# An FFT convolution followed by two MLPs: the second half of a scratch buffer read back in two partition ranges on two queues, and one product moved ahead

## The reference

```python
X = np.fft.rfft(x, axis=1)                 # x: (2, 3008, 256) float32
Y = X * (filt_r + 1j * filt_i)[None]
y = np.fft.irfft(Y, n=3008, axis=1)        # tokens: 2 * 3008 = 6016 rows of 256
h = y.reshape(6016, 256) @ w1_in           # 256 -> 2048
z = np.maximum(0.01 * h, h) @ w1_out       # 2048 -> 256
h = z @ w2_in
r = np.maximum(h, 0.0)
out = (r * r) @ w2_out                     # (6016, 256)
```

## Time and profile before

| | us |
|---|---|
| median of 3 runs | 1065.8 (1065.09 to 1067.39) |
| the profiled execution's own time | 1064.64 |
| its span | 1062.5 |
| PE busy | 1057.0 |
| DVE busy | 827.9 |
| ACT busy | 563.3 |
| POOL busy | 316.1 |

### The profile page before, as it was taken

One profiled execution on the slowest core, in us unless ns is written; L12 is line 12 of the kernel. 1 busy time (PEld: TensorE's weight loads), 2 busy tenths in 40 slices (PEclk: granted clock), 3 DMA queues, 4 the chain that ended last, 5 costly groups with the idle time before them and its releaser, 6 DMA issues.

```text
span 1062.5 us, 13988 instructions
## 1 busy us (share of the span) xinstructions
PE 1057.0 (99%) x5120; PEld 879.8 (83%) x5120; DVE 827.9 (78%) x1142; ACT 563.3 (53%) x979; POOL 316.1 (30%) x287
## 2 busy tenths in 40 slices
PE   9999999999999999999999999999999999999998
PEld 9558888888888888888999888888888888888998
DVE  2877898887887887787887886887887887786666
ACT  3667564564554654555554554644554554454543
POOL 1995654434343343341321211220220220210000
PEclk9999999999999999999999999999999999999999
DMA  9696000121112112112344000100100100100100
GB/s 316 176 304 231 10 1 17 36 52 46 51 49 49 52 47 51 52 33 55 118 152 147 21 1 1 40 1 1 40 1 1 40 1 1 40 1 1 40 1 35
DMA packets 66724, 61.45 MB, mean 58 GB/s; under 512 B 40688, under 2 KB 53856, under 8 KB 66656
## 3 DMA queue, kind: packets, MB, share of 16 engines
q1 hardware_dynamic: 66160, 60.06, 18.2%
q10 hardware_dynamic: 496, 0.49, 0.1%
HBM read 36.55 MB, written 23.99 MB: 57 GB/s over the span
## 4 chain that ended last, share of the span: by engine, by line
PE 98%; DMA 1%; SPq 0%; DVE 0%; ACT 0%; issue 0%; ACTq 0%
PE PS L1046 16%; PE PS L1047 16%; PE PS L1048 16%; PE PS L1054 14%; PE PS L1055 14%; PE PS L1056 14%; PE PS L935 2%; PE PS L959 2%; PE PS L1002 1%; PE PS L1022 1%; PE PS L979 1%; DMA X<-in_x 0%; DMA zu<-U 0%; DMA V<-zu 0%; SPq L219 0%; PE PS L999 0%
## 5 line engine op out<-in xcount | busy, mean ns | idle before, releaser
L683 ACT ACTIVATE GH<-GF 128x512 fp32r<-128x512 f32 (+1 forms) x384 | 238.7, 622 | 295.3 <-DVE GF L878 154.4
L884 DVE TENSOR_TENSOR GL<-GF,GH 128x512 fp32r<-128x512 f32 (+1 forms) x384 | 273.7, 715 | 110.4 <-ACT GH L683 103.7
L1048 PE MATMUL PS<-GH,WOL 128*128 128x512 f32 (+1 forms) x768 | 295.8, 385 | 0.0
L1047 PE MATMUL PS<-GL,WOH 128*128 128x512 f32 (+1 forms) x768 | 295.8, 385 | 0.0
L1046 PE MATMUL PS<-GH,WOH 128*128 128x512 f32 (+1 forms) x768 | 295.8, 385 | 0.0
L1054 PE MATMUL PS<-XH,WIH 128*128 128x512 f32 (+1 forms) x672 | 259.5, 386 | 0.0
L1056 PE MATMUL PS<-XH,WIL 128*128 128x512 f32 (+1 forms) x672 | 258.8, 385 | 0.0
L876 DVE SCALAR_TENSOR_TENSOR GF<-GF 128x512 f32<-128x512 f32 (+1 forms) x192 | 167.5, 913 | 1.6
L1048 PEld LDWEIGHTS PS<-GH,WOL 128*128 128x128 f32 x768 | 144.2, 188 | 27.0
L1046 PEld LDWEIGHTS PS<-GH,WOH 128*128 128x128 f32 x768 | 144.2, 188 | 26.8
L1047 PEld LDWEIGHTS PS<-GL,WOH 128*128 128x128 f32 x768 | 144.2, 188 | 26.6
(11 more groups left out here) (85 smaller groups left out, 941.9 us busy)
## 6 DMA issues: line engine op xcount, KB each, us to landing
V<-zu SPq DMA_DIRECT2D x12, 512.0 KB, 5.9
zu<-U SPq DMA_DIRECT2D x31, 192.0 KB, 3.7
out_y<-YT SPq DMA_DIRECT2D x5, 1024.0 KB, 4.3
X<-in_x SPq DMA_DIRECT2D x8, 512.0 KB, 8.9
FL<-in_filt SPq DMA_DIRECT2D x16, 224.0 KB, 5.0
wi<-PWH SPq DMA_DIRECT2D x16, 224.0 KB, 2.5
wi<-PWL SPq DMA_DIRECT2D x16, 224.0 KB, 3.1
WIH<-wi SPq DMA_DIRECT2D x8, 448.0 KB, 3.4
```

The lines of the kernel that those rows point to most:

```text
L683: nc.scalar.activation(GH[:, g, 0:width(s)], GF[:, g, 0:width(s)], ACT.Copy).then_inc(g_hi[kind], 1)
L884: nc.vector.tensor_tensor(GL[:, g, 0:w], GF[:, g, 0:w], GH[:, g, 0:w].bitcast(f32), ALU.subtract).then_inc(g_lo[kind], 1)
L1047: nc.tensor.matmul(acc, wh, xl, start=False, stop=False)
L1048: return nc.tensor.matmul(acc, wl, xh, start=False, stop=last)
```

## The change

The reads of V[0] stay as they are. The six reads of V[1] become six others, over three pieces of 4, 8 and 12 residues. Partitions 0 to 95 of each piece (the "body"; frequencies of units 8 to 13) are read by ACT's queue, from a place behind `y_copy(4)` and `x_round0(1)`, once units 11, 12 and 13 are stored. Partitions 96 to 127 (the "rest"; units 14 and 15) are read by SP's queue behind the last three stores, where the six reads stood. Sequences 12 and on wait for both parts of their piece: 12 and 13 for the first, 14 to 17 for the second, 18 to 23 for the third. And `up_1(1)` moves from behind `up_5(0)` to the place behind `up_1(0)`, in front of sequence 12.

```diff
+V_PIECES = ((0, 4), (4, 12), (12, 24))
+V_BODY = 96
...
+            def load_v_rest(n):
+                a, b = V_PIECES[n]
+                by_js = zu[1].rearrange("j s m e -> (j s) m e")
+                sp.dma_start(V[1][V_BODY:, a:b, :, :].rearrange("p m b d -> p m (b d)"), by_js[V_BODY:, a:b, :]).then_inc(v_rest[n], 16)
...
             for n in range(UNITS - RINGS, UNITS):
                 sp.wait_ge(*stored(n))
-            for g in range(MH // 4):
-                load_v(1, g)
+            for n in range(len(V_PIECES)):
+                load_v_rest(n)
...
+            def load_v_body(n):
+                a, b = V_PIECES[n]
+                by_js = zu[1].rearrange("j s m e -> (j s) m e")
+                act.dma_start(V[1][0:V_BODY, a:b, :, :].rearrange("p m b d -> p m (b d)"), by_js[0:V_BODY, a:b, :]).then_inc(v_body[n], 16)
+
             for c in Y_ACT:
                 if DRAIN[-1] <= c < 14:
                     y_copy(c)
                 if c == 4:
                     x_round0(1)
+                    for n in range(UNITS - 2 - RINGS, UNITS - 2):
+                        act.wait_ge(z_out[n % RINGS], 32 * (n // RINGS + 1))
+                    for n in range(len(V_PIECES)):
+                        load_v_body(n)
...
-                pe.wait_ge(v_in[half][g], 16)
+                if half == 0:
+                    pe.wait_ge(v_in[g], 16)
+                else:
+                    piece = [a <= 4 * g < b for a, b in V_PIECES].index(True)
+                    pe.wait_ge(v_body[piece], 16)
+                    pe.wait_ge(v_rest[piece], 16)
...
             up_1(0)
+            up_1(1)
             for c in range(CH, 19):
                 sequence(c)
...
             for s in range(1, SLOTS):
-                up_1(s)
-                if s == 1:
+                if s > 1:
+                    up_1(s)
+                else:
                     sequence(22)
                 up_2(s)
```

More of the change, by code:

```diff
@@ L117, in fft_mlp_kernel @@
         z_out = [sem(f"z_out{r}") for r in range(RINGS)]
-        v_in = [[sem(f"v_in{h}{g}") for g in range(MH // 4)] for h in range(2)]
+        v_in = [sem(f"v_in{g}") for g in range(MH // 4)]
+        v_body = [sem(f"v_body{n}") for n in range(len(V_PIECES))]
+        v_rest = [sem(f"v_rest{n}") for n in range(len(V_PIECES))]
         y_ps = sem("y_ps")
@@ L249, in stored, with load_v @@
                 return z_out[i % RINGS], 32 * (i // RINGS + 1)
[L251 to L254, removed]
+            def load_v(g):
+                by_js = zu[0].rearrange("j s m e -> (j s) m e")
+                sp.dma_start(V[0][:, 4 * g:4 * g + 4, :, :].rearrange("p m b d -> p m (b d)"),
+                             by_js[:, 4 * g:4 * g + 4, :]).then_inc(v_in[g], 16)
+            def load_v_rest(n):
+                a, b = V_PIECES[n]
+                by_js = zu[1].rearrange("j s m e -> (j s) m e")
+                sp.dma_start(V[1][V_BODY:, a:b, :, :].rearrange("p m b d -> p m (b d)"), by_js[V_BODY:, a:b, :]).then_inc(v_rest[n], 16)
             for b in range(B):
@@ L277, in _ @@
                 if 0 <= i - NU < MH // 4:
-                    load_v(0, i - NU)
+                    load_v(i - NU)
             for n in range(UNITS - RINGS, UNITS):
                 sp.wait_ge(*stored(n))
-            for g in range(MH // 4):
-                load_v(1, g)
+            for n in range(len(V_PIECES)):
+                load_v_rest(n)
             sp.wait_ge(p_ps, 4 * UNITS)
```

## The result

Median of six runs 1073.05 us (1071.83 to 1075.51) against 1065.44 before (1064.16 to 1067.39, six runs): ratio 1.0072, 95% interval [1.006, 1.0083]. The change costs 7.6 us where "no difference" was forecast, and lies outside the range. The profiled execution took 1074.45 around a span of 1072.3.

A forecast was written before the change was run, and what follows sets the result against it. PE was taken to bound the kernel, with one 1.33 us hole before sequence 12. 1.33 - 0.05 = 1.3 us gained from the median of 1065.8 gave 1064.5 us, range 1063.3 to 1066.8.

The forecast's parts named there:

- What bounds the kernel, and the size of the hole: PE holds 98% of the span; its one wait, before sequence 12 for V, is 1.33 us, all this edit can bring.
- Edit 1: up_1(1) in front of sequence 12 runs inside the hole: worth 0.70 us even if V comes no sooner.
- Edit 2a: First rest on SP behind the last stores: lands 2.7 us after issue (2.1 to 3.84), at 85.6, before 86.14.
- Edit 2b: Body on ACT, issued at 80.00, delays the stores in SP's queue by 0 to 0.8 us, taken as 0.1.
- Edit 2c: Three body issues in ACT's queue take 1.43 us and free ACT 0.96 late; no cost to PE.
- Edit 2d: Third piece of V, wanted by sequence 18 at 91.5, lands at 91.0 to 91.9: no wait, above 0.4 us.
- ACT held up: Rival: three slow issues free ACT at 85.6, delaying y_copy(6) and up_2(0); time 1066.5 us, chance 0.09.
- What is late next: Behind the hole, up_7(1) waits 0 to 0.1 us for whole_c(0), taken as 0.05; no other PE wait.
- The rule: Skill's advice against splitting by partition halves, since transfers serialize: V would land no sooner, at 86.72, gain 0.70 us.
- Only the order counts: Rival: the first rest comes as late as the old piece, V at 86.7; gain 0.7, time 1065.1, chance 0.26.
- The slow one: Rival: third piece lands at 93 to 95, sequence 18 waits 1.5 to 3.5 us; 1067.5 at 94.5, chance 0.13.

The follow-up runs named there:

- e4: Changed kernel with V[1] in six pieces of four residues, only the first split between ACT and SP, the others whole on SP; ratio to before 0.9987.
- e11: The same kernel as e4, measured once more on another chip: 1063.91 us against 1065.36, ratio 0.9982.
- e6: Kernel before with up_1(1) in front of sequence 12 and each SP read of V[1] cut in 96 and 32 partitions; ratio to before 1.0009.
- e2: Changed kernel without the body: SP reads all 128 partitions of the three pieces behind the last stores; ratio to before 1.0005.
- e3: Changed kernel with six pieces of four residues in place of three, body on ACT, rest on SP; ratio to before 1.0057.
- e5: Five foreign reads: kernel before with up_1(1) moved, ACT also reading five times 512 KB into an unused tile; ratio to before 1.0056.
- e9: Kernel before with up_1(1) moved and each SP read of V[1] cut by residues, three and one, all 128 partitions; ratio to before 0.9991.

## Why the prediction was wrong, step by step

**What bounds the kernel, and the size of the hole: right.** The kernels without a hole (e4, e11) gained 1.44 in the seam: the 1.33, and 0.11 within sequences 12 to 18 (6.16 where they took 6.27).

**Edit 1: right as far as it can be told.** 0.55 in the seam and 0.6 in the median for 0.70 forecast, with an interval that takes in 1.

**Edit 2a, the rest on SP: wrong, and this decided it.** "Below, it takes 2.1 us ... above, 3.84": it took 10.5. The upper bound was a row in which no other queue had work, and the one row with two queues at work was read as a rule: "they took turns". In the earlier trace rows both queues' stores had been issued within 0.01 us of each other. A read that SP issued behind a large backlog of ACT's had no turn for 2 to 6 us. The five foreign reads show that with whole partitions and small rows. The trace of before held a warning that I did not look for. ACT's last store was issued at 78.48, behind some 1 MB that SP had issued from 74.9 on. The kernel before, the DMA queues from 78.5 to 80 us:

```profile
DMA packets 358, 0.50 MB, mean 331 GB/s; under 512 B 29, under 2 KB 306, under 8 KB 358
...
q1 hardware_dynamic: 358, 0.50, 97.4%
```

Not one packet of q10 for 1.5 us, where V's first read, on empty queues, had packets within about 1 us of its issue at 82.88. It is a weak warning, 0.6 us.

**Edit 2b: right.** The last stores landed 0.3 later (84.48 - 79.75 = 4.73 against 82.88 - 78.47 = 4.41), within 0 to 0.8. Not even this is the body's for sure: without one, the same stores took 4.33 (e6) to 4.70 (e2).

**Edit 2c, ACT's queue: right in what came of it, not in the price.** Three issues held it for 2.3 us, from 80.30 to 82.68, where the sum took 1.43 and the rival "ACT held up" about 2.5; both lie within 0.9 to 5.6. They began 1.53 us after the start of sequence 4, where I had 2.51, while `y_copy(4)` was still running. It cost nothing: `up_1(0)` started 7.17 after sequence 4 as before, and the last rounding waited 0.95 for POOL as before.

**Edit 2d, the rate: wrong.** "From 81.5 to 83.8 the body moves 870 of its 2304 KB" took the full 380 KB in a us from whole partitions. ACT's queue moved 0.34 MB from 83 to 84 us, but from 84 to 90 it ran at 180 to 270 GB/s, and this is what made the backlog long: at the full rate 2304 KB from 81.5 are through at 87.6, while in the change packets of q10 still fill the engines at 90. The third piece itself caused no wait (the last rest landed at 85.3 + 14.7 = 100.0), but only since sequence 12 was so late.

**What is late next: right** where it could be seen: e4 has no wait of PE behind the hole.

**The clock: left out.** With an idle time of 7.5 us TensorE dropped to 1.2 GHz, 2.1 us more. None of my cases held an idle time of more than 4 us.

**The rule.** The Trainium skill's "don't bother" for disjoint partition halves (page "DMA: Bandwidth & Descriptors", section "Rules for kernel authors") was nearer than I made it, yet both of us had the price wrong: the rule says the parts serialize, and the trace shows them slower than one whole read (249 and 239 GB/s against 386). And it isn't always right: with the first piece alone the cut gains 0.9 in the seam over the order alone, and in the runs made side by side 0.5 in the median (1063.92 against 1064.40).

**The rivals.** "Only the order counts" had the late rest, with a wait of 0.6 us where it was 7.7. The slow one had its place at the third piece; it was at the first. A rest behind the body was considered only by turns. The range was worked from one mechanism with one rate.

What of the 8.5 us belongs to what: the order gave -0.55; the same change without the large pieces (e3) lengthens the seam by 6.3; the large pieces add 2.2 (e2 priced them at 1.0 alone, and the difference isn't explained). Split partitions alone are +1.6 over the order (e6), held-back reads alone +5.3 (e5, with a clock drop of its own). The parts don't add up to the whole; the likely reason, which no run shows by itself, is that the slow rate makes the backlog last longer.

## What to carry to other kernels

A transfer that must be quick when its data are ready should not be issued behind another engine's backlog: what is put early on a second queue must be through by then, so put there only as much as fits into the idle time of the DMA engines (384 KB here, and one of 512 KB did no harm either), not all that could be read. Before a read is cut by partitions, price it at the rate of the cut, not at that of the whole; cut by columns (here by residues) if it must be cut. And any wait that could reach several us has a second price in TensorE's clock: it fell to 0.50 in the profiles with holes of 4.3, 4.7 and 7.5 us.

## What the runs showed of the hardware that I had not expected

- A DMA issued by SP while ACT's queue had 1.8 to 2.2 MB left to move had no packet moved for 3.5 to 6.3 us (e5, e3, the change); in the earlier trace rows, with one store in each queue, packets alternated.
- Reads of HBM to 96 and 32, or 64 and 64, partitions ran at 249 and 239 GB/s, reads to 128 partitions at 359 (e9, rows of 1 and 3 KB), 386 (before, 4 KB) and 426 (e2, 12 KB).
- Rows of 12 KB went as single packets at 426 GB/s on whole partitions (e2).
- ACT issued a DMA while its activation before it was still in work (80.30, within 80.17 to 80.77), and before the start of the next activation (80.67), which stands ahead of the DMA in the program.
